# Loading the resident weights late instead of evenly in an attention and mixture-of-experts kernel

## What is computed

```python
scores = q @ k.T / sqrt(D) + bias              # masked outside 0 <= i - j < 128
attn = exp(scores - max) / (sum + 1e-9)
x = (attn @ v) as rows of tokens               # [2304, 512]
logits = x @ w_gate                            # 8 experts, 288 tokens each
# highest logit first: a token goes to the expert, if both are free
out[mask] = relu(x[mask] @ w1[e]) @ w2[e]      # for each expert e
h = out @ w_in                                 # [512, 2048]
result = (h * sigmoid(h)) @ w_out              # [2048, 512]
```

## Time and profile before

| | |
|---|---|
| median of 3 runs | 855.27 us (853.61 to 867.32) |
| profiled execution, its own time | 851.91 us |
| its span | 850.0 us |
| TensorE busy | 820.5 us, 97% |
| DVE, ScalarE, POOL busy | 485.4, 331.5, 304.7 us |
| end of the attention part (barrier passed) | 168.28 us |

### The profile page before, as it was taken

One profiled execution on the slowest core, in us unless ns is written; L12 is line 12 of the kernel. 1 busy time (PEld: TensorE's weight loads), 2 busy tenths in 40 slices (PEclk: granted clock), 3 DMA queues, 4 the chain that ended last, 5 costly groups with the idle time before them and its releaser, 6 DMA issues.

```text
span 850.0 us, 17955 instructions
## 1 busy us (share of the span) xinstructions
PE 820.5 (97%) x6903; PEld 743.3 (87%) x6903; DVE 485.4 (57%) x1561; ACT 331.5 (39%) x767; POOL 304.7 (36%) x336
## 2 busy tenths in 40 slices
PE   9999999749999999999999999999999999999997
PEld 7888778638888998998899889988998999899996
DVE  7778677777655665565565343756665475642111
ACT  4666566504224333432433224333432433343221
POOL 1133343704236234433522344234323623433223
PEclk9999999959999999999999999999999999999999
DMA  9789988315012404310440031204302130430000
GB/s 127 141 174 183 169 183 199 124 53 162 14 59 70 125 1 128 89 38 10 119 125 2 6 122 57 80 2 128 112 14 79 61 113 1 128 100 25 1 1 37
DMA packets 149764, 71.43 MB, mean 84 GB/s; under 512 B 98736, under 2 KB 136112, under 8 KB 149680
## 3 DMA queue, kind: packets, MB, share of 16 engines
q1 hardware_dynamic: 144336, 60.56, 29.3%
q0 software_dynamic: 2976, 9.44, 3.5%
q10 hardware_dynamic: 2368, 0.30, 0.3%
HBM read 60.83 MB, written 9.44 MB: 83 GB/s over the span
## 4 chain that ended last, share of the span: by engine, by line
PE 76%; DVE 2%; POOL 1%; issue 1%; DMA 0%; ACT 0%; POOLq 0%; DVEq 0%; ACTq 0%
PE hp L1228 12%; PE hp L1229 12%; PE hp L1230 12%; PE acc L1313 8%; PE acc L1315 8%; PE acc L1314 8%; PE acc L1228 4%; PE acc L1230 4%; PE acc L1229 4%; PE rt L1180 2%; PE rt L1195 1%; DVE test L1476 0%; PE acc L1222 0%; DMA x_rows_sb<-x_rows,tokens 0%; DVE wa_l L1635 0%
## 5 line engine op out<-in xcount | busy, mean ns | idle before, releaser
L1156 POOL TENSOR_TENSOR h_l<-h_raw,h_h 128x256 fp32r<-128x256 f32 (+1 forms) x128 | 115.5, 903 | 264.4 <-ACT h_h L1437 264.2
L1706 DVE TENSOR_TENSOR h_raw<-hp,gate 128x256 f32<-128x256 f32 (+1 forms) x128 | 58.6, 458 | 179.8 <-ACT gate L1429 178.8
L1228 PE MATMUL hp<-xy_h,res_h 128*128 128x256 f32 (+1 forms) x512 | 154.0, 301 | 0.0
L1229 PE MATMUL hp<-xy_l,res_h 128*128 128x256 f32 (+1 forms) x512 | 151.4, 296 | 0.0
L1230 PE MATMUL hp<-xy_h,res_l 128*128 128x256 f32 (+1 forms) x512 | 151.2, 295 | 0.0
L1144 POOL TENSOR_TENSOR wb_l<-wb_raw,wb_h 128x512 fp32r<-128x512 f32 x64 | 85.4, 1336 | 127.0 <-ACT wb_h L1373 127.0
L1429 ACT ACTIVATE gate<-hp 128x256 f32<-128x256 f32 (+1 forms) x128 | 52.7, 412 | 195.3 <-PE hp L1230 193.6
L1313 PE MATMUL acc<-res_h,h_h 128*128 128x512 f32 x288 | 116.7, 405 | 0.0
L1315 PE MATMUL acc<-res_h,h_l 128*128 128x512 f32 x288 | 113.5, 394 | 0.0
L1314 PE MATMUL acc<-res_l,h_h 128*128 128x512 f32 x288 | 113.5, 394 | 0.0
L1228 PEld LDWEIGHTS hp<-xy_h,res_h 128*128 128x128 f32 x512 | 96.5, 188 | 3.6
(11 more groups left out here) (235 smaller groups left out, 1673.9 us busy)
## 6 DMA issues: line engine op xcount, KB each, us to landing
wa_raw<-in_moe_w_dram SPq DMA_DIRECT2D x64, 256.0 KB, 3.5
wb_raw<-in_moe_w_dram SPq DMA_DIRECT2D x64, 256.0 KB, 3.2
k_rows<-in_k_dram SPq DMA_DIRECT2D x64, 72.0 KB, 4.3
q_rows<-in_q_dram SPq DMA_DIRECT2D x60, 72.0 KB, 3.0
v_rows<-in_v_dram SPq DMA_DIRECT2D x32, 128.0 KB, 2.7
stage<-in_moe_w_in_dram SPq DMA_DIRECT2D x8, 512.0 KB, 5.0
x_rows<-x_rows_sb SPq DMA_DIRECT2D x8, 512.0 KB, 3.2
stage<-in_moe_w_out_dram SPq DMA_DIRECT2D x8, 512.0 KB, 4.4
```

The lines of the kernel that those rows point to most:

```text
L1156: pool.tensor_tensor(h_l[:, cols], h_raw[:, cols], h_h[:, cols].bitcast(FP32), ALU.subtract).then_inc(g_low, 1)
L1228: nc.tensor.matmul(out_, weights_h, cols_h, start=start, stop=False)
L1229: nc.tensor.matmul(out_, weights_h, cols_l, start=False, stop=False)
L1706: nc.vector.tensor_tensor(h_raw[:, h_cols(s, f)], hp[(A_NO[s, f] - 1) % 2][:, 0:width], gate[:, 0:width], ALU.mult).then_inc(g_done, 1)
```

## The change

A table `PIECES` says how many pieces are loaded behind step g, where it was one in each. They now stand at the end of the step, behind the keys and queries and behind the store. Steps 0 and 1 have none, steps 2, 4, 6, 8, 9 and 10 one each, step 11 two, steps 12 and 13 three each, step 14 two. The ranking step 2 becomes two: `key` stays at (3,1) and `first_thresholds` moves to (3,3). Lines of the kernel after stand up to five further down.

```diff
+PIECES = [0, 0, 1, 0, 1, 0, 1, 0, 1, 1, 1, 2, 3, 3, 2, 0]
             for g in range(NG):
                 if g + 3 < NG:
                     load_values(g + 3)
-                stage_piece(g)
                 if g + 5 < NG:
                     load_rows(g + 5)
                 if g % 2:
                     store_x(g)
+                for n in range(sum(PIECES[:g]), sum(PIECES[:g + 1])):
+                    stage_piece(n)
...
                 elif part == 1:
                     number()
+                elif part == 2:
+                    key()
                 else:
-                    key()
                     first_thresholds(b)
...
                     elif (g % PAIRS, kind) == (3, 1):
                         rank_batch(b, 2)
+                    elif (g % PAIRS, kind) == (3, 3):
+                        rank_batch(b, 3)
...
-            for part in range(3):
+            for part in range(4):
                 rank_batch(B - 1, part)
```

## The result

The kernel after takes 858.36 us (median of 8 runs, 856.62 to 859.42), the kernel before 854.44 us in the median of its 8. The ratio is 1.0075 (95% interval 1.0055 to 1.0095): slower by 6.4 us, which is within 2%. The medians lie only 3.9 us apart because that of before counts two executions in a slower state (867.32 and 902.81 us), which the ratio leaves out. The forecast was 860 us, some 6.6 us over before.

The account below looks back on a forecast made before the run. TensorE is busy 97%; attention loses 3.35 us to late stores and DVE sets its exit. That gain lies inside the exit's 6.6 us delay: 851.91 + 6.6 = 858.5, by the median 861.9; forecast 860, range 854.0 to 868.

Parts of the forecast that it names:

- What bounds: Attention part before: late x-row stores cost pairs 4 to 11 3.35 us; DVE sets the barrier exit, POOL has 4.1 us spare.
- Early pieces: Steps before 11: fewer weight pieces ahead of the stores remove every stall, gaining 3.35 us; pair 11 ends at 125.0.
- SP at step 11: SP reaches step 11 at 127.2, earlier by five pieces' transfers, 9.3 us.
- The tail: From step 11: ten pieces left, one per 4.0 us on POOL, ending at 174.6; barrier exit 174.9, 6.6 us later.
- early bound: Best case for the late pieces: SP at step 11 at 125.0, POOL without a gap, exit 170.4, +2.1 us.
- The ranking split: Comparison with first thresholds moved to slot (3,3) on DVE: taken as 0, bounds −0.4 to +0.4 us per batch.
- POOL beside DVE: Last batch's ranking: POOL's splits may slow four steps by 1.0 us each, DVE's end 168.6, hidden, no term.
- B: Rival, not slower: attention shrinks by 5.4 us, exit at 168.3 or earlier, 852 to 855 us; chance 0.08 with its variant.
- Its variant: The exit doesn't wait for POOL: gain 3.35 us, 848.6 to 852 us; chance within the 0.08 of B.
- C: Rival, longer tail: SP saves only 0.64 us a piece, exit +12.7 us, 864.6 us, 868 by the median; chance 0.15.
- D: Rival: TensorE's clock returns late after the ranking, costing 10 us more, 868.5 us, 872 by the median; chance 0.05.
- sum by the profiled execution: Total forecast: 851.91 us of the profiled execution before plus 6.6 us, 858.5 us.

Follow-up runs that it names:

- table alone: Kernel after with the last ranking step in one part as before, pieces still by the new table; 859.18 us, ratio 1.0046 to before.
- twelve late: Kernel after with two more pieces late: four by step 10, then three behind each of steps 11 to 14; 865.18 us, ratio 1.0159 to before.
- ones behind the store: Kernel after with one piece in every step, 0 to 15, at the step's end behind loads and store; 854.16 us, ratio 0.9975 to before.
- behind the loads: Kernel before with each step's piece behind key and query loads, ahead of the store, ranking split; run twice: 849.67 us (0.9979), 848.74 us (0.9968).
- nine early: Kernel after with one piece behind each of steps 2 to 10, then 2, 2, 2, 1; 850.93 us, ratio 0.9930 to before.
- ten early: Kernel after with one piece behind each of steps 1 to 10, then 2, 2, 1, 1; 848.39 us, ratio 0.9965 to before.

## Why the prediction was right

What bounds. It said that 3.35 us are lost to stores of x rows that SP issues late, and that the exit hangs on DVE with POOL 4.1 us behind. Both held: the seven pairs take 65.4 us after, and the barrier has followed POOL in every kernel whose POOL was last (after, table alone, twelve late, ones behind the store) and DVE in the others.

Early pieces. All stalls gone, pair 11 forecast at 125.0, measured 125.63 with a start 0.66 us later. The result is right, the reason was only part of it. The working priced each removed piece at its transfer, 1.76 us; with the same number of pieces and another place (ones behind the store) the stalls go as well. The place ahead of the loads, which the working did not name, is a cause that suffices alone; whether the removed pieces would suffice too is open.

SP at step 11: forecast 127.2 by five pieces' transfers, 9.3 us, measured 125.86, 10.6 us earlier than before. The number is near, the reason doesn't hold. With all eleven pieces still ahead of step 11, only placed behind the loads, SP is there at 130.35, 131.24 and 131.68 (ones behind the store, and behind the loads twice), so the place alone gives 4.8 to 6.2 us, and the five pieces taken away give the other 4.5 to 5.8 us, 0.9 to 1.2 us a piece and not the 1.85 of the working. They could hardly give more: SP had caught up and waited for the ends of pairs 9 and 10, and the earliest it can be at step 11 is some 0.4 us ahead of pair 11's end, as with twelve late. The pieces gave less than reckoned, and the place, which was left out, made up for it: that is luck.

The tail. Piece 6 on POOL from 134.6, measured 135.10; 4.0 us a piece, measured 4.01; end 174.6, measured 175.19; exit 174.9, measured 175.50. Piece 5 was forecast for 130.8 and came at 130.80. Here two errors cancel: SP issued piece 5 at 125.33, 1.3 us earlier than forecast, and 5.5 us passed to its first cast instead of 4.2. For piece 6 it is the same: issued at 128.75 and not 130.0, but 6.35 us passed to its first cast. The 4.2 us came from a stretch with the queue at 54%. So the early bound was out of reach as worked out: with twelve late SP was at step 11 as early as can be, and 5.6 us passed from the issue of the next piece to its first cast. The sum of 6.6 us stands against 7.2 us in the profiles and 6.4 us in the runs.

The ranking split. Forecast at nothing; the run of it alone shows 0.9991 (0.9961 to 1.0020), and the seven pairs take 65.4 us with it and without it.

POOL beside DVE. The working let the last ranking grow by at most 4 us, to 168.6; it grew by 3.2 and ended at 168.01, hidden under POOL's tail. The rule of the Trainium skill (SBUF — State Buffer, Who interferes with whom) is borne out in its selection too: steps with two SBUF inputs are stretched by up to a POOL instruction's length (1.23 us at 163.96 against 0.20), the reductions are not, and at 167.64 DVE was first and the split lost 0.2 us. It costs nothing in the kernel after, and 2.2 us in the kernel with nine early, where DVE sets the exit.

The rivals. B needed a faster pace than 9.23 us a pair; in none of the nine experiments do the seven pairs from 4 to 11 take less than 65.4 us. Its variant needed an exit that doesn't wait for POOL; it came 0.31 us behind POOL's end in four kernels. C needed SP at step 11 at 133; it was at 126. D, the clock: the part behind the barrier kept its length to 0.2 us; the table alone has 1.8 us more in its one profile, with a second dip of the clock, a fraction of the 10 us that D needed.

The number. 860.0 lies 1.6 us over the measured 858.36. It was set between the sum by the profiled execution, 858.5, and that by the median of three runs, 861.9. The sum by the profiled execution was the better: 858.36 / 1.0075 = 852.0 us stand behind the measured ratio, and the profiled execution had 851.91.

## What to carry to other kernels

Work that is moved late to free a shared queue ends up behind somebody: before moving it, count the pieces left, times the time per piece of the slowest stage of their chain, against the time left to the next barrier. Here ten pieces at 4.0 us, 40 us, stood against the 33 us from 135.10, where POOL began them, to 168.28, where the barrier had been.

Look at the place within a step before thinning the steps out. One large transfer a step ahead of eight small ones on one queue cost the pairs 3.4 us in the kernel before; behind them and behind the store it cost them nothing, with the same bytes in the same steps.

When one chain is shortened until another sets the end, look at what the two share: POOL's splits still slowed the ranking on DVE when they were no longer the last thing.

## What was not expected of the hardware

A high share of the DMA engines over a stretch didn't mean that the stores were late. In 80 to 100 it is 0.98 before, 0.93 with ones behind the store and 1.00 in the kernel after, and in the last two no store is waited for. The order on the queue decided.

The kernel before scatters more than the ones without stalls: in the rounds with ten early, 20 of its 21 executions lay between 848.91 and 859.35 us, and the 11 of the one with the piece behind the loads between 848.24 and 852.29. No trace was kept of a late execution, so the cause is open.
